# Row sums guarded one block later, GpSimd's weight copies behind its scatters, and two counts of unread products, in an attention and mixture-of-experts kernel

## The reference

```python
mask = (rel >= 0) & (rel < window)                      # window 128
scores = np.where(mask, scale * q @ k.T + bias, -1e9)
attn = np.exp(scores - max); attn = attn / (np.sum(attn, -1) + 1e-09)
x = (attn @ v)                                           # 1152 x 512
...
logits = x @ w_gate                                      # 1152 x 8
expert_idx = argmax(logits); gate_w = softmax(logits)[expert_idx]
disp[e, counts[e]] = x[i]                                # first come, capacity 288
h = relu(disp @ w1); y = h @ w2                          # 8 experts, 512 -> 1024 -> 512
out[i] = gate_w[i] * y[expert_idx[i], pos[i]]
...
h = x @ w_in; g = h * sigmoid(h); return g @ w_out       # 512 -> 2048 -> 512
```

## Time and profile before

| | us |
|---|---|
| median of 3 runs | 470.24 |
| the 3 runs | 470.24, 471.21, 462.97 |
| the profiled execution | 465.1 |
| its span, first to last instruction | 463.3 |
| TensorE busy | 441.1 (95%) |
| VectorE busy | 231.7 (50%) |
| ScalarE busy | 222.1 (48%) |
| GpSimd busy | 236.6 (51%) |

### The profile page before, as it was taken

How to read it: one execution, slowest core, us unless ns; L and a number is a source line. 1 busy time by engine, 2 the same in 40 slices (tenths; PEclk the granted TensorE clock), 3 DMA queues, 4 the chain that set the end, 5 groups by cost and what they waited for, 6 DMA issues and landing times.

```text
span 463.3 us, 8375 instructions
## 1 busy us (share of the span) xinstructions
PE 441.1 (95%) x2939; PEld 400.1 (86%) x2939; DVE 231.7 (50%) x711; ACT 222.1 (48%) x549; POOL 236.6 (51%) x170
## 2 busy tenths in 40 slices
PE   5899999979999999999999999999999999999993
PEld 4677777758999999999999999998999988999982
DVE  4578887766674866857755342132322131312230
ACT  4877778633685666675677643122222221221220
POOL 3006788741989899999999996602000002000002
PEclk9999999858999999999999999999999999999998
DMA  9999960028968697697898500001000001000002
GB/s 177 272 275 254 313 192 12 25 89 288 377 208 262 226 317 256 209 303 282 234 280 301 184 1 1 0 2 45 23 0 0 0 0 68 0 0 0 0 0 74
DMA packets 54567, 64.29 MB, mean 139 GB/s; under 512 B 32096, under 2 KB 32096, under 8 KB 54528
## 3 DMA queue, kind: packets, MB, share of 16 engines
q1 hardware_dynamic: 52752, 59.08, 41.5%
q0 software_dynamic: 1776, 4.73, 2.8%
HBM read 54.35 MB, written 9.44 MB: 138 GB/s over the span
## 4 chain that ended last, share of the span: by engine, by line
PE 79%; DVE 9%; ACT 7%; issue 2%; DMA 1%; POOL 0%; DVEq 0%; POOLq 0%
PE bank L1175 14%; PE bank L1176 14%; PE bank L1177 14%; PE bank L1202 14%; PE bank L1201 6%; PE bank L1049 3%; ACT prob L570 3%; DVE w_lo L971 3%; PE bank L1089 3%; PE bank L1199 3%; PE bank L1066 2%; ACT w_hi L600 2%; PE bank L1033 1%; PE bank L1200 1%; DVE bank L936 1%
## 5 line engine op out<-in xcount | busy, mean ns | idle before, releaser
L459 POOL TENSOR_TENSOR w_lo<-w_raw,w_hi 128x1024 fp32r<-128x1024 f32 x72 | 179.2, 2522 | 22.9 <-ACT w_hi L600 19.6
L1000 DVE TENSOR_TENSOR g_full<-bank,sigmoid 128x384 f32<-128x384 f32 x48 | 26.8, 558 | 131.8 <-ACT sigmoid L686 126.7
L541 POOL DMA_INDIRECT out_dram<-out_stage,permcol x9 | 8.8, 972 | 150.8 <-ACT out_stage L706 147.5
L686 ACT ACTIVATE sigmoid<-bank 128x384 f32<-128x384 f32 x48 | 23.6, 492 | 125.1 <-PE bank L1177 116.4
L600 ACT ACTIVATE w_hi<-w_raw 128x1024 fp32r<-128x1024 f32 x74 | 77.8, 1053 | 0.0
L936 DVE TENSOR_REDUCE bank<-bank 128x192 f32<-128x384 f32 (+5 forms) x96 | 49.1, 512 | 38.4 <-PE bank L1202 38.3
L1175 PE MATMUL bank<-x_hi,w_hi 128*128 x192 | 64.9, 338 | 0.0
L1177 PE MATMUL bank<-x_hi,w_lo 128*128 x192 | 64.6, 336 | 0.0
L1176 PE MATMUL bank<-x_lo,w_hi 128*128 x192 | 64.5, 336 | 0.0
L1202 PE MATMUL bank<-hidden,w_hi 128*128 128x384 f32 (+5 forms) x224 | 63.1, 351 | 0.0
L1175 PE MATMUL bank<-w_hi,g_hi 128*128 128x512 f32 x144 | 56.7, 394 | 0.8 <-DVE g_lo L1004 0.8
(11 more groups left out here) (139 smaller groups left out, 794.3 us busy)
## 6 DMA issues: line engine op xcount, KB each, us to landing
w_raw<-in_moe_w_dram SPq DMA_DIRECT2D x64, 512.0 KB, 5.5
dispatch_dram<-zeros SPq DMA_DIRECT2D x4, 1152.0 KB, 7.7
w_raw<-in_moe_w_in_dram SPq DMA_DIRECT2D x8, 512.0 KB, 5.5
w_raw<-in_moe_w_out_dram SPq DMA_DIRECT2D x8, 512.0 KB, 7.1
dispatched<-dispatch_dram SPq DMA_DIRECT2D x9, 384.0 KB, 8.0
q_raw<-in_q_dram SPq DMA_DIRECT2D x8, 256.0 KB, 5.3
k_raw<-in_k_dram SPq DMA_DIRECT2D x8, 256.0 KB, 5.5
v_raw<-in_v_dram SPq DMA_DIRECT2D x8, 256.0 KB, 5.6
```

Of the source, the lines that this page charges most:

```text
L459: nc.gpsimd.tensor_tensor(wlo[s][:, sl], raw[s][:, sl], whi[s][:, sl], ALU.subtract).then_inc(pool_lo, 1)
L686: nc.scalar.activation(sig[:, f % 2, :], bank[f % 4][:, 0:TB], ACT.Sigmoid).then_inc(sig_ready, 1)
L1000: nc.vector.tensor_tensor(gf[:, f % 2, :], bank[f % 4][:, 0:TB], sig[:, f % 2, :], ALU.mult).then_inc(gf_ready, 1)
```

## The change

Three things are changed. First, `sums_guarded` and `sums_inverted` leave the end of the block. `sums_guarded` of tile t-2 now stands in block t behind the first two heads' scores and ahead of `take_pT`, and `sums_inverted` stands between `take_pT` and `normalize`. The row sums are kept one block longer, so they have three buffers in place of two. Second, GpSimd's CAST for the eighth n stands behind the scatter of tile n; it stood behind `slots` of tile n+1. Third, `WARM` goes from (6, 12) to (8, 13).

```diff
-    WARM = (6, 12)
+    WARM = (8, 13)
...
-    rsum, o = at("row_sum", [P, 2, H], F32, o)
+    rsum, o = at("row_sum", [P, 3, H], F32, o)
...
                 if 1 <= t <= EARLY:
-                    high_here(t - 1)
-
                     pool.wait_ge(seen_ready, t + 2)
                     low_here((t - 1) // PIECES, (t - 1) % PIECES, t)
...
                                              bounds_check=E * C - 1, oob_is_err=False).then_inc(scattered, 16)
+                if t < EARLY:
+                    high_here(t)
...
-                                         accum_out=rsum[0:r, t % 2, h:h + 1]).then_inc(probs_ready, 1)
+                                         accum_out=rsum[0:r, t % 3, h:h + 1]).then_inc(probs_ready, 1)
...
-                start(nc.vector.tensor_scalar_add(rsum1[0:r, :], rsum[0:r, t % 2, :], 1e-9))
+                start(nc.vector.tensor_scalar_add(rsum1[0:r, :], rsum[0:r, t % 3, :], 1e-9))
...
                 scores(u, 0)
                 if t == 2:
                     dve.wait_ge(consts, 1)
+                if t >= 2:
+                    sums_guarded(t - 2)
                 if t >= 1:
                     take_pT(u - 1)
                 if t >= 2:
+                    sums_inverted(t - 2)
                     normalize(t - 2)
                 scores(u, 1)
...
                 take_pT(u - 1)
-                if t >= 1:
-                    sums_guarded(t - 1)
-                    sums_inverted(t - 1)
+            sums_guarded(NTOK - 2)
             place_found(NTOK - 3)
+            sums_inverted(NTOK - 2)
             gate_found(NTOK - 3)
```

## The result

| | us |
|---|---|
| changed kernel, 4 runs | 474.58, 468.81, 474.33, 467.69; median 471.57 |
| kernel before, 4 runs | 470.24, 471.21, 462.97, 466.76; median 468.50 |
| ratio | 1.0145, 95% interval 1.0089 to 1.0201 |
| the profiled execution | 474.58 (before 465.1) |

The changed kernel is slower, by 1.45% or 6.8 us, where the forecast had 2.5 us. Medians take all runs, while the ratio leaves out slow executions, those more than 1.5% above the fastest of the same kernel: here 470.24 and 471.21 of the kernel before, so that its base is 464.9 and not 468.50, while the changed kernel's 474.58, 1.47% above its fastest, stays in. Between the medians of all eight lie 3.1 us. The time, 471.6, lies in the range given; the change by the ratio is nearly three times the one forecast.

A forecast was written before the change was run, and what follows sets the result against it. TensorE was taken to bound the experts fully and to be nearest its limit in the block loop. Terms 0 + 1.7 + 1.1 - 0.6 + 0 + 0.3 = +2.5 us gave 469.9 at the mean level, range 462.5 to 475.5.

The forecast's parts named there:

- Removing the guard from the block's end: Block loop, VectorE: taking L766 from its old place gains 0, -0.3 at most, since TensorE's scores are awaited anyway.
- The reciprocal in the chain: Block loop: L771 between L760 and L779 starts L779 0.23 later, lengthening TensorE's waits; +1.7 us, from 0 to 3.4.
- The stall at the new place: Block 5, VectorE: L766 waits for GpSimd's L498 ahead of L760, once only; +1.1 us, from 0.3 to 1.33.
- L766 is caught in every block: Rival, block loop: a 1.33 us stall in each of 8 blocks, +12.0 in sum, 479.4 at the mean; chance 0.06.
- The CASTs: Block loop, GpSimd: earlier CASTs remove the stall of L805 in block 9; -0.6 us, from -1.4 to 0.
- The products before the branch: Ahead of the branch, TensorE: two more unread products are covered by the plan; cost 0 to 0.1.
- behind it: Behind the branch, TensorE: a thirteenth unread product, last thing waited for, adds its length; +0.3 us.
- The rival's full clock: Rival, around the branch: thirteen products at full clock gain 1.4, stalls vanish; sum -2.0 to -2.8; chance 0.28.
- The level: Whole kernel: base moved from the profiled 465.1 to the runs' mean 467.4, by +2.3.

The follow-up runs named there:

- row sums alone: Kernel before with only the row-sum edit (three buffers, guard ahead of the copy, reciprocal ahead of normalize): 466.03, ratio 1.0014.
- no guard: Changed kernel with L766 left out, the 1e-9 not added and the reciprocal reading the row sums directly: 466.08, ratio 1.0010 against the kernel before.
- guard back: Changed kernel with L766 back at the end of the block before, all else as changed: 466.05, ratio 1.0028 against the kernel before.
- the next two: Changed kernel timed again, median 469.92, ratio 1.0068; and changed kernel with WARM back at (6, 12), 467.85, ratio 1.0062.
- the second trace of the changed kernel: Profiled execution from timing the unaltered changed kernel again: 12 runs, median 469.92 against 465.88, ratio 1.0068.
- fewer products: Kernel before with CASTs behind the scatters and WARM = (8, 8), row sums untouched: 465.93, ratio 1.0000.
- the reduction in the guard's place: Changed kernel with a tensor_reduce copying the row sums instead of L766's addition, 1e-9 left out: 468.17, ratio 1.0057 against the kernel before.
- the CASTs alone: Kernel before with only the CASTs moved behind the scatters: 465.47, ratio 0.9971.
- the products alone: Kernel before with only WARM changed from (6, 12) to (8, 13): 466.40, ratio 0.9995.

## Why the prediction was wrong, point by point

**Removing the guard from the block's end, 0.** Right within the measurement: 1.0004 (-1.2 to +1.5 us) with it left out altogether. Nothing speaks against the reason given, that a stall of up to 1.33 us lay in VectorE's wait for the scores.

**The reciprocal in the chain, +1.7.** The mechanism is there: TensorE's waits for x_tile went from 1.2 to 4.0 us wherever the reciprocal had moved and the guard wasn't held (row sums alone, no guard, guard back). The size holds inside the loop, 1.8 to 2.2 us from block 2 to block 9. What the sum lacked is that part of it comes back behind block 9, 1.3 to 1.8 us in the same traces, as the table shows. The runs of the three kernels stand at +0.65, +0.5 and +1.3 us (1.0014, 1.0010 and 1.0028 of 466), none of them clear of 0.

**The stall at the new place, one hit of +1.1, and no second.** This step failed, though not in the price of a hit: one cost 1.04 us. That the two agree is luck, since the 1.1 was reckoned for a wait behind L498 and the 1.04 is that of a CAST behind a scatter. The step failed in the number of hits, and in that nothing was set down for the clock. I reckoned that, once held, VectorE would be late against GpSimd, and the guard would fall behind the instruction that had held it from then on. But GpSimd doesn't run on: its low part waits for `seen_ready`, which comes from L811, and L811 stands behind the guard in VectorE's program. When the guard is held, GpSimd is held as well (the 11.2 us above), the two keep their step, and the next block can meet in the same way: four blocks of eight in one trace, two and one in the next two. It can, but need not: with one hold, in block 8, the next guard came at 84.70 and its scatter at 85.01. That the semaphore is what brings the meeting back is read from the traces; no kernel without that wait was run. It was not the L498 of the prediction either but the scatter with the CAST behind it; behind L498 the longest guard that I find at its new place took 0.30 (at 56.81 in the second trace of the changed kernel). And a hold can be followed by a stretch of halved clock on TensorE, for which the sum had no term: 2.9 of the 9.0 us with four holds, 2.0 of the 6.0 with two, by the estimate above. The step priced the two edits one by one and let only a lateness pass from one to the other; in truth the second edit put a CAST where the first had put the guard. The rival "L766 is caught in every block" had the repetition, though behind L459 or L498, and got 6 in 100, on the same wrong ground, that VectorE's delay moves it out of the way.

**The CASTs, -0.6.** Alone -1.4 (-2.9 to +0.3) by the ratio and -0.3 by the medians, with fewer products 0. Neither shown nor refuted. The long L805 and L808 of blocks 7 and 9 are gone from the changed kernel's trace (0.23 each), as forecast; in the changed kernel the same CASTs are what holds the guard.

**The products before the branch, 0; behind it, +0.3.** Right within the measurement: -0.2 us (-1.8 to +1.3) for both. With 8 the pause before the second group shrank from 2.10 to 1.15. The thirteen took 4.75 us in the changed kernel's trace, less than the twelve before, since the clock rose earlier among them; TensorE turned the rows 1.1 us behind their arrival (116.16), where it was 1.4 before. So the products were still the last thing waited for, as forecast. The rival's full clock came in some executions.

**The level.** I put the base at 467.4, the mean of four executions. With some thirty runs the kernel before has a median of 465.8 to 466.4, and the changed one, in twelve, 469.9, which happens to be the forecast's number: a base too high by 1.5 and a change too small by as much. It is no merit of the sum.

What stays open: how much of the loss in the runs is the guard's hold. For the hold: the loss needs guard and moved CAST together, the loop grows with the number of guards held, and one hold has a price of its own. Against its being all: the reduction in the guard's place, short in its one profile, was 0.57% slower in its runs, and the clock's stretches come without a hold too. Which of them the slower runs had, only their traces could say.

## What to carry to other kernels

A tiny VectorE instruction that waits for GpSimd's long ones is harmless behind the last thing that others wait for, and dear ahead of it; before moving it, lay GpSimd's program beside the new place, and take the program as it will be after all the other edits. Ask of each delay whether the engine that caused it is waiting, by some semaphore, for the one that it delayed: if so, the two stay in step and the delay can come back in any round. And price edits that touch the same meeting point together: here one cost nothing, the other perhaps gained, and both lost 3 to 7 us. Last, a term for a delay is not complete with its own length: see what the clock of the engine that waits does behind it, and take more than one trace, since here the same program lost or gained 2 us from one to the next.

## What the runs showed of the hardware that I had not expected

**The hold begins before the CAST's recorded start.** At 41.68 in the changed kernel the guard stood 0.75 us before the CAST began by the trace, and at 75.46 in the second trace 0.36, both times while the scatter was still running. With a scatter alone the guard took 0.16 at 39.41 and 0.33 at 75.44 in the kernel with the row sums alone, where it ended at 75.77, just before the scatter did (75.81). The Trainium skill, page "SBUF — State Buffer", section "Who interferes with whom", has the rule that whichever of the two issues first gets the shared ports for the whole instruction. The trace agrees that the CAST kept them to its end (43.48 and the guard's 43.52), but by the recorded starts the guard was first. The rule would still hold if a ready CAST counted as issued while the scatter ahead of it runs; no run here tests that.

**GpSimd's L498 lets VectorE in halfway.** This instruction (L496 in some kernels) takes 1.59 us, and the rule of the Trainium skill just named isn't borne out by it. A guard that began 1.1 to 1.4 us after its start was held to its end, but one that began 0.1 to 0.5 after it ended 0.70 to 0.73 after the start, in nine cases in five kernels, and two that began 0.76 and 0.80 after it passed in 0.15 and 0.16. GpSimd's recorded spans are rough, yet the nine ends agree within 0.03. With the CASTs alone:

```profile
80.07 0.55 DVE L766 TENSOR_SCALAR row_sum<-row_sum 128x8 f32<-128x8 f32 x1
...
79.91 1.59 POOL L496 TENSOR_SCALAR x_gated<-x_tile,gate 128x512 f32<-128x512 f32 x1
```

The guard was over at 80.62, and L496 ran on until 81.50. The prediction's +1.1 counted on the guard at 47.30 waiting for an L498 that would run until about 48.4, that is from about 46.8; by these rows a guard 0.5 behind its start would have been through at about 47.5.

**An instruction with two inputs in SBUF was held as well.** In the kernel with the row sums alone, L811, a TENSOR_TENSOR of 128x8 that takes 0.17, took 0.89 across a CAST that ran from 60.05 to 61.09:

```profile
60.22 0.89 DVE L811 TENSOR_TENSOR seen<-seen,onehot 128x8 fp32r<-128x8 f32 x1
```

**One small instruction can be held for ten microseconds.** One execution of the kernel with the products alone took 476.61 us. Its block loop was like that of before; the loss is at the start of the dense layer. VectorE's timeline:

```profile
259.81 0.56 DVE L1000 TENSOR_TENSOR g_full<-bank,sigmoid 128x384 f32<-128x384 f32 x1 [1.55 <-ACT sigmoid L686]
260.29 9.83 DVE L1004 TENSOR_TENSOR g_lo<-g_full,g_hi 128x384 fp32r<-128x384 f32 x1
270.25 0.56 DVE L1000 TENSOR_TENSOR g_full<-bank,sigmoid 128x384 f32<-128x384 f32 x1
```

and GpSimd's, the last seven of a row of eleven low parts without a gap:

```profile
253.33 16.37 POOL L459 TENSOR_TENSOR w_lo<-w_raw,w_hi 128x1024 fp32r<-128x1024 f32 x7
```

An instruction of 0.55 us with two inputs in SBUF began at 260.29 and ended at 270.12, behind the end of GpSimd's whole row at 269.70; though it had waited all along, it didn't come in between any two of the last four. TensorE stood still for nine microseconds, from 261.4 to 270.3, and its clock was halved for ten. The longest L1004 of the traces of before and of the changed kernel took 2.02 and 2.03. This part of the program is the one of the kernel before, so a loss of 10 us stands ready in it that one execution meets and another doesn't. Single executions of the kernel before and of seven others lie at 476 us and more without any such reason in their edit, so it is the first thing that I would look at next; whether they are of this kind, only their traces could say.
